# Mixture-of-experts kernel: 128-row tiles of one expert become two 64-row halves with an expert each, on two column tiles, in native fp32

## What is computed

```python
x = attn_out.transpose(0, 2, 1, 3).reshape(1152, 512)
# layer 0: 8 experts, w1[e] 512 x 1024, w2[e] 1024 x 512
expert_idx = argmax(x @ w_gate, 1); gate_w = softmax(...)[expert_idx]
y = gate_w * (relu(x @ w1[e]) @ w2[e])     # rows beyond the capacity of 288: zero
# layer 1: the same with weights of its own, for rows with y @ w_skip > 0
out = y.copy(); out[active] = y[active] + gate2_w * (relu(y @ w1[e]) @ w2[e])
```

## Times and profile before

| | |
|---|---|
| median of 3 executions | 707.31 us (703.5 to 710.21) |
| the profiled execution's own time | 709.03 us |
| its span | 707.3 us |
| PE busy | 640.4 us (91%) |
| PE weight loads busy | 453.4 us (64%) |
| DVE / ACT / POOL busy | 295.6 / 262.5 / 232.3 us |
| chain that ended last, by engine | PE 84%, DMA 4%, DVE 4% |

### The profile page before, as it was taken

How to read it: one execution, slowest core, us unless ns; L and a number is a source line. 1 busy time by engine, 2 the same in 40 slices (tenths; PEclk the granted TensorE clock), 3 DMA queues, 4 the chain that set the end, 5 groups by cost and what they waited for, 6 DMA issues and landing times.

```text
span 707.3 us, 11546 instructions
## 1 busy us (share of the span) xinstructions
PE 640.4 (91%) x3400; PEld 453.4 (64%) x3401; DVE 295.6 (42%) x501; ACT 262.5 (37%) x434; POOL 232.3 (33%) x211
## 2 busy tenths in 40 slices
PE   3759999999999999479999999999758999999984
PEld 3647877777777877356666766666456666566641
DVE  5426565666666574755303330120075654400000
ACT  4525565656565565222322322322202222222320
POOL 4173470825436830011211121121110444343332
PEclk9979999999999999789999999999959999999996
DMA  4786527163453104489912986140049999512110
GB/s 100 169 280 137 126 65 151 51 133 85 98 133 68 33 0 137 139 330 416 403 41 85 294 310 228 50 158 21 28 151 346 405 354 321 201 45 73 33 59 23
DMA packets 43446, 111.00 MB, mean 157 GB/s; under 512 B 16516, under 2 KB 16516, under 8 KB 42480
## 3 DMA queue, kind: packets, MB, share of 16 engines
q1 hardware_dynamic: 38384, 96.67, 43.3%
q0 software_dynamic: 5040, 14.06, 5.9%
HBM read 102.16 MB, written 13.37 MB: 163 GB/s over the span
## 4 chain that ended last, share of the span: by engine, by line
PE 84%; DMA 4%; DVE 4%; issue 3%; POOL 2%; ACT 2%; SPq 1%; ACTq 0%; POOLq 0%; DVEq 0%
PE psum L951 23%; PE psum L906 13%; PE psum L682 12%; PE psum L696 10%; PE psum L730 8%; PE psum L914 6%; PE psum L882 4%; PE psum L758 2%; DMA qraw<-in_q_dram 2%; PE psum L936 1%; DMA xraw<-moe_in,rows_in 1%; PE psum L742 1%; DMA wsecond<-in_moe_w_dram 1%; PE psum L887 1%; PE psum L726 1%
## 5 line engine op out<-in xcount | busy, mean ns | idle before, releaser
L951 PE MATMUL psum<-wsecond,HT 128*128 x384 | 175.8, 602 | 5.2 <-ACT HT L1119 4.6
L1182 DVE TENSOR_SCALAR_CACHE_REDUCE probs<-psum 128x1152 f32<-128x1152 f32 x72 | 97.6, 1357 | 75.2 <-PE psum L682 75.2
L951 PEld LDWEIGHTS psum<-wsecond,HT 128*128 128x128 f32 x384 | 72.1, 193 | 84.3 <-issue 83.4
L682 PE MATMUL psum<-KT,QT 128*128 128x384 f32 x480 | 106.6, 363 | 20.5 <-DVE KT L1289 9.8
L996 ACT ACTIVATE probs<-probs,nmax 128x1152 f32<-128x1152 f32 x72 | 90.7, 1260 | 48.3 <-DVE probs L1182 48.3
L682 PEld LDWEIGHTS psum<-KT,QT 128*128 128x128 f32 x480 | 84.9, 198 | 31.8 <-issue 16.6
L1339 DVE CAST wring<-wraw 128x1024 f32 (+1 forms) x56 | 39.9, 728 | 144.5 <-PE psum L914 136.3
L906 PE MATMUL psum<-wring,XTh 128*128 x384 | 98.2, 409 | 1.9 <-ACT XTh L1106 1.9
L696 PE MATMUL psum<-ident,probs 128*128 128x128 f32 x648 | 82.7, 276 | 3.3 <-ACT probs L996 2.8
L906 PEld LDWEIGHTS psum<-wring,XTh 128*128 128x128 f32 x384 | 72.5, 194 | 18.5 <-issue 2.8
L696 PEld LDWEIGHTS psum<-ident,probs 128*128 128x128 f32 x648 | 73.6, 142 | 11.5 <-issue 3.7
(11 more groups left out here) (163 smaller groups left out, 619.5 us busy)
## 6 DMA issues: line engine op xcount, KB each, us to landing
wraw<-in_moe_w_dram SPq DMA_DIRECT2D x64, 512.0 KB, 6.6
wsecond<-in_moe_w_dram SPq DMA_DIRECT2D x64, 512.0 KB, 7.8
qraw<-in_q_dram SPq DMA_DIRECT2D x30, 288.0 KB, 7.2
kraw<-in_k_dram SPq DMA_DIRECT2D x14, 576.0 KB, 7.2
V<-in_v_dram SPq DMA_DIRECT2D x8, 576.0 KB, 3.8
moe_in<-zero SPq DMA_DIRECT2D x9, 256.0 KB, 3.0
out_dram<-moe_in SPq DMA_DIRECT2D x1, 2304.0 KB, 9.6
moe_in<-xpair SPq DMA_DIRECT2D x16, 128.0 KB, 2.0
```

The source lines that it names most:

```text
L682: mm = pe.matmul(dst, QT[par][:, piece, q0:q0 + P], KT[par][:, b * S + c * KB:b * S + (c + 1) * KB], start=(i == 0), stop=(i == 2 * len(pa ...
L951: mm = pe.matmul(bank(Y_BANK), HT[:, c * P:(c + 1) * P], w, start=(c == 0), stop=(c == FC - 1), skip_group_check=True)
L1182: nc.vector.tensor_scalar(probs[:, t, :].rearrange("p (c k) -> p c k", c=3), scores_in(h, t), -SCALE, None, ALU.mult, ALU.min, accum_out=n ...
```

## The change

- **Tiles.** The unit is a grain of 64 rows (`GRAIN`); a tile is two grains, each with an expert of its own (`tab_grain`, one entry per grain). Experts begin on 64-row borders. `NSLOT`, the largest number of tiles, goes from 16 to 14.
- **Products.** `product` issues two matmuls with 64-column stationaries: the left grain into psum rows 0 to 63, moving the weights out of the ring, and the right grain into rows 64 to 127, moving a copy of its weights out of `wright`. Both products are native fp32. The cuts of W1 and X, `by_hi`, `by_lo`, `rest_of_x` and `cut_expert` go.
- **Copies.** `fill_right` copies the right grain's weights, 4 parts of 128 x 1024, for every tile: W1 on ACT, between relu(t) and the XT copy of tile t+1; W2 on DVE, right after `copy_y`.
- **Rings.** W1 4 experts, W2 3 experts (`RINGS`). SP's loop now issues W2 of expert a and then W1 of expert a+1, both waiting for the tiles of expert a-3: W2 for `y_done`, W1 for `hidden_done`.
- **Results.** The gate goes into relu's scale. DVE instead of ACT evacuates y; in layer 1 it adds the residual in the same instruction, so that it waits for `res_loaded` there, and `load_residual(t)` waits for `y_copied` of t-1. The logits of layer 1 are made by DVE, nine multiply-and-add reductions over 512 columns per tile with output to psum; only the last tile's go over PE as before.
- XT and HT are copied in halves; the constants of the subtraction go; three attention buffers move so that the rings fit; `wnext` (gate rows, broadcast to 128 partitions) is loaded once.

```diff
-    RING, RING2 = 2, 4
+    NTAB = NSLOT * PER_TILE
+    RINGS = (4, 3)
...
+        def fill_right(eng, copy, k, m, t, filled):
+            place = t * PER_TILE + 1
...
+            expert = eng.value_load(tab_grain[m][0:1, at], min_val=0, max_val=E - 1)
+            slot = eng.snap(ring_slot(k, m, expert))
+            for part in range(PARTS):
+                eng.wait_ge(w_loaded[k][part], expert * 16 + (E * m + 1) * 16)
+                copy(wright[k][:, part * PIECE:(part + 1) * PIECE],
+                     piece_of(k, slot, part).rearrange("p o f -> p (o f)")).then_inc(filled, 1)
...
+            def other_experts(m):
+                with sp.Fori(RINGS[1], E - 1) as a:
+                    load_second(m, a, m, a - RINGS[1])
+                    load_first(m, a + 1, m, a - RINGS[1])
+                load_second(m, E - 1, m, E - 1 - RINGS[1])
...
                 def load_residual(t, count):
+                    wait(pool, y_copied, t)
...
+                def product(k, lhs, b, c, cols, slot, first, last):
+                    left = wring[k][:, bass.ds(slot, 1), cols].rearrange("p o f -> p (o f)")
+                    pe.matmul(psum[0:GRAIN, b, :], lhs[:, c * P:c * P + GRAIN], left, start=first, stop=last,
+                              skip_group_check=True)
+                    return pe.matmul(psum[GRAIN:P, b, :], lhs[:, c * P + GRAIN:(c + 1) * P], wright[k][:, cols],
+                                     start=first, stop=last, skip_group_check=True)
...
-                def step(t, first=False, second=False):
-                    ring = first_weights(t)
-                    pe.wait_ge(xt_ready, t + 1)
-                    by_hi(XTh, (HID_BANK, HID_BANK + 1), DC, F, ring)
...
-                    by_lo(XTl, (HID_BANK, HID_BANK + 1), DC, F, ring).then_inc(hidden_done, 1)
+                def step(t, first=False):
+                    hidden_product(t)
+                    if first:
+                        pe.wait_ge(gates_found, m + 1)
+                    else:
+                        y_product(t - 1)
                     turn_x(t + 1)
...
-                        next_logits(t - 2)
                     turn_hidden(t)
...
+                def step(t):
                     relu(t)
+                    act.wait_ge(hidden_done, t + (START + 1))
+                    fill_right(act, nc.scalar.copy, FIRST, m, t + 1, w1_right_[m])
                     copy_xt(t + 1)
+                    copy_hidden(t)
...
+            def copy_y(m, t):
+                dve.wait_ge(y_done_[m], t + (START + 1))
+                wait(dve, y_stored_[m], t * 16)
+                if m == 0:
+                    nc.vector.tensor_copy(ysb[:], bank(Y_BANK)).then_inc(y_copied_[m], 1)
+                else:
+                    dve.wait_ge(res_loaded, 16 * t + 16)
+                    nc.vector.tensor_tensor(orow[:], bank(Y_BANK), res[:], ALU.add).then_inc(y_copied_[m], 1)
+            def next_logits(t):
+                dve.wait_ge(y_copied_[0], t + 1)
+                for e in range(E + 1):
...
+                    nc.vector.tensor_tensor_reduce(out=bank((YT_BANK, LG_BANK)[e % 2]), in0=ysb[:], in1=wnext[:, e, :], scale=1.0, scalar=0.0,
+                                                   op0=ALU.mult, op1=ALU.add, accum_out=lrow[:, e:e + 1]
+                                                   ).then_inc(lrow_ready, 1)
...
+                def step(t):
+                    copy_y(m, t)
+                    fill_right(dve, nc.vector.tensor_copy, SECOND, m, t + 1, w2_right_[m])
+                    if m == 0:
...
+                        next_logits(t)
```

More of the change, by code:

```diff
@@ new lines, in hidden_product @@
+                def hidden_product(t):
+                    expert = left_expert(t)
+                    slot = pe.snap(ring_slot(FIRST, m, expert))
+                    wait(pe, relu_ready, t)
+                    for c in range(DC):
+                        pe.wait_ge(w_loaded[FIRST][c], expert * 16 + (E * m + 1) * 16)
+                        pe.wait_ge(w1_right_[m], PARTS * t + (c + 1))
+                        if c % 2 == 0:
+                            pe.wait_ge(xt_ready, 2 * t + (1 + c // 2))
+                        for i in range(F // 512):
+                            mm = product(FIRST, XT, HID_BANK + i, c, slice(c * F + i * 512, c * F + (i + 1) * 512), slot,
+                                         c == 0, c == DC - 1)
+                    mm.then_inc(hidden_done, 1)
@@ new lines, in y_product @@
+                def y_product(t):
+                    expert = left_expert(t)
+                    slot = pe.snap(ring_slot(SECOND, m, expert))
+                    wait(pe, y_copied, t)
+                    for c in range(FC):
+                        part = c // (FC // PARTS)
+                        if c % (FC // PARTS) == 0:
+                            pe.wait_ge(w_loaded[SECOND][part], expert * 16 + (E * m + 1) * 16)
+                            pe.wait_ge(w2_right_[m], PARTS * t + (part + 1))
+                        if c % (FC // 2) == 0:
+                            pe.wait_ge(ht_ready, 2 * t + (1 + c // (FC // 2)))
+                        mm = product(SECOND, HT, Y_BANK, c, slice(c * DM, (c + 1) * DM), slot, c == 0, c == FC - 1)
+                    mm.then_inc(y_done, 1)
@@ L977, in _ @@
                 turn_x(0)
                 step(0, first=True)
-                step(1, second=True)
+                step(1)
                 with pe.Fori(2, NSLOT) as t:
@@ L1129, in copy_yt @@
-                def copy_yt(t):
-                    act.wait_ge(y_turned, t + 1)
-                    nc.scalar.copy(yT[:], bank(YT_BANK)).then_inc(yt_ready, 1)
-                def copy_logits(t):
-                    act.wait_ge(lg_done, t + 1)
-                    at = slice(t, t + 1) if isinstance(t, int) else bass.ds(t, 1)
-                    nc.scalar.copy(logits2[:, at, :].rearrange("p o c -> p (o c)"), bank(LG_BANK, E + 1)
-                                   ).then_inc(lg_copied, 1)
-                def step(t, first=False, second=False):
-                    if not first:
-                        copy_hidden(t - 1)
+                    for i in range(2):
+                        act.wait_ge(hid_turned, 2 * t + (i + 1))
+                        if i == 0:
+                            wait(act, y_done_[m], START + t)
+                        nc.scalar.copy(HT[:, i * 512:(i + 1) * 512], bank(HT_BANK + i)).then_inc(ht_ready, 1)
```

423 lines of the change are left out of this document (152 added, 271 removed).

## The result

| | before | after |
|---|---|---|
| median | 708.76 us (703.5 to 710.69, 4 executions) | 719.95 us (718.86 to 721.92, 4 executions) |
| ratio, with 95% interval | 1 | 1.0152 (1.0115 to 1.0188) |
| span of the profiled execution | 707.3 us | 717.1 us (its own time 718.86) |

What follows compares the result with a forecast made beforehand. PE was taken to bound both tile loops. Layer 0 -39.9, routing +0.3, layer 1 +31.6 and tail -2.6 summed to -10.6 on 707.3, so 697 us; own range 683 to 711, wider 672 to 716.

Steps and rivals of the forecast that it cites:

- the price of the waits in layer 1: Layer 1's late W1 loads put at 33.6 us and late residual gathers at 14.9, giving layer 1 199.6 us, +31.6.
- The tile on PE: Both tile loops: 10 and 9 tiles, 15.2 us of PE per step, each pair of passes 0.43 us.
- column tiles don't overlap: Rival in the tile products: paired passes lack full overlap, 13.7 us more per tile, 958 us; chance 0.06.
- The logit reductions: DVE's nine per tile, put at 0.8 us each, 7.2 us; DVE 11.1 of 15.2 us per tile, hidden.
- that rival (718 us): DVE becomes the bound of layer 0, from 1.25 us per reduction, 718 us at 1.44; chance 0.12.
- Layer 0: The first layer's tile loop: 166.5 us against 206.4, a gain of 39.9 us.
- Weights late in layer 1: W1 of experts 5 and 6 13.8 us late ahead of tiles 3 and 4, plus 3.0 clock each: 33.6 us.
- the weights come in time: Rival in layer 1: W1 loads of experts 5 and 6 not late, 33.6 us go, 663 us; chance 0.12.
- Residual late: Layer 1: DVE's copy_y waits for the residual gather, with W2's fill behind it; 14.9 us in all.
- The total: Whole span: -39.9 + 0.3 + 31.6 - 2.6 = -10.6 us on 707.3, so 697 us.
- Everything in layer 1 a bit worse: Rival of worse clock and gathers in layer 1, counted inside the forecast's own range, without a chance of its own.

Runs made afterwards that it cites:

- the short loops: e7 with the tile loops of PE, ACT, DVE and POOL ending at these inputs' 10 and 9 tiles: 641.7 us, ratio 0.9064 to the kernel before.
- e6: e3 with ACT copying XT of tile 1 before filling W1's right half in each layer's first step: 649.09 us, ratio 0.914 to the kernel before.
- e2: Changed kernel with POOL gathering the residual one step earlier, behind the store of tile t-1: 693.29 us, ratio 0.9777 to the kernel before.
- e3: Changed kernel with both edits, W1 issued before W2 and the residual gathered a step earlier: 658.28 us, ratio 0.9292 to the kernel before.
- e5: Changed kernel with DVE only copying y out in layer 1 and POOL adding the residual, gather as late as before: 699.03 us (one execution).
- e7: e6 with SP issuing W1 loads one expert further ahead, W1 of a+2 before W2 of a: 646.27 us, ratio 0.9087 to the kernel before.
- e1: Changed kernel with SP issuing W1 of expert a+1 before W2 of expert a: 695.47 us, ratio 0.9812 to the kernel before.
- e8: e3 with experts beginning on 128-row borders again, 13 and 11 tiles, both halves of a tile the same expert: 729.11 us (one execution).
- e4: Changed kernel, same load order, with W2 of experts 3 to 6 of layer 1 loaded by half: 714.56 us (one execution).

## Why the prediction was wrong

The step that failed is the price of the waits in layer 1. The waits that were named are the ones that came, but W1 late by 13.8 us was 16.7 and 17.2, the gathers put at 14.9 us in all took 19.8, and the lower clock behind a gather's wait, which the working put at nothing without a reason, took 4.3 more. Layer 1 came out at 215.6 us and not 199.6, and that is 16.0 of the 20.4 us by which the span was missed.

**The tile on PE: right.** 10 and 9 tiles. A pair of passes starts every 0.43 us, 32 pairs in a row, and a step takes 352.36 - 337.01 = 15.35 us, against 15.2. PE's timeline in after, layer 0, one step:

```profile
337.01 0.64 PE L887 MATMUL psum<-w1ring,XT 128*64 x1
337.02 0.64 PE L889 MATMUL psum<-wright,XT 128*64 128x512 f32 x1
337.50 0.59 PE L887 MATMUL psum<-w1ring,XT 128*64 x1
...
337.92 0.59 PE L887 MATMUL psum<-w1ring,XT 128*64 x1
...
343.93 0.59 PE L887 MATMUL psum<-w2ring,HT 128*64 x1
```

The left and the right half start within 0.01 us of each other. First product 6.92, y product 6.87, turns 1.56: of the 1.48 that I had put for turns and for going in and out of column tiles, 0.08 were missing. The rival "column tiles don't overlap" (958 us) is out; attention's rows were a sound basis for 64 passes in a row. The Trainium skill (TensorEngine Tiling (Array Packing), Key Properties) says that a change of tiling mode drains TensorE. The trace doesn't show a drain by itself, but it bounds the price: the turns of 128 x 128 between the products, with a change of mode on either side, take 1.56 us, against 0.44 + 0.79 of the earlier trace rows.

**DVE: right.** The logit reductions, in after, layer 0:

```profile
462.96 0.14 DVE L1281 DVE_READ_ACCUMULATOR2_ANT lrow<- 128x1 f32 x1
462.96 0.73 DVE L1281 CUSTOM_DVE_ANT_0 psum<-ysb,wnext 128x512 f32<-128x512 f32 x1
...
468.42 0.17 DVE L1286 COPY logits<-lrow 128x9 f32 x1
471.03 0.69 DVE L1271 COPY ysb<-psum 128x512 f32<-128x512 f32 x1 [2.43 <-issue]
```

0.73 us each and one every 0.65, under the 0.8 taken and far from the 1.25 at which that rival (718 us) decides. Its 718 is near the measured time, by luck: DVE is busy for 85.75 of the 169.90 us of layer 0.

**Layer 0: the mechanism right, 3.4 us short.** The first product has 9.15 us instead of 8.4 (+0.75); the gap to tile 1 is 5.9, not 5.5 (+0.4), but the clock costs 1.6 there, not 3.0 (-1.4); steps and the gap ahead of y(9) +1.0; from the end of y(9) to the routing 6.9 instead of 4.2 (+2.7). The last is a step that the working left out: DVE leaves its loop only after the skipped tiles, and copies y(9) 2.9 us after it is done, where 0.7 was put. With the short loops it is 0.97 us.

**Weights late in layer 1: right in place and cause, too small.** Two gaps, ahead of tiles 3 and 4, released by ACT's copies waiting for W1, just as named. The order of SP's loop removed both and the bytes hardly mattered, so the rival "the weights come in time" (663 us) is out. The term that was mis-sized is the wait: 13.8 us each were put, 16.7 and 17.2 measured (+6.3 in all). At tile 3, SP asks 0.9 us after y(1) ends (0.3 was put), the last part is copied 15.7 us after SP's first issue (13.6 was put for bytes, landing, gathers and store), and 1.7 us lie from there to the first pass (1.45 was put). The clock took 2.3 and 2.0 instead of 3.0 each (-1.7).

**Residual late: right in kind, too small.** The experiments with an early gather and with POOL's addition both removed it. Put were 14.9 us: y(1) 5.0, y(4) 2.5, y(5) to y(7) 0.9 each, y(8) 4.7. Measured: 6.1, 3.7, 1.4 to 1.5 each, and for y(8) 0.8 more than the gap that the working gave it (10.0 against 9.2), so 19.8: +4.9. The failed part is that these waits cost clock too: +2.6 at y(1) and +1.7 at y(4). I had counted the clock for the 14 us gaps and for the loop ends only, though the row of an idle time of 3.08 us with its 3 us of loss was in hand. A wait of 3.6 or 5.9 us should have had the same surcharge.

The sum for layer 1: W1 gaps +6.3 and -1.7, gathers +4.9 and +4.3, eight steps +1.2, the gap to tile 1 +0.6, together +15.6 of the +16.0 measured.

**The total.** -39.9 for layer 0 against +31.6 for layer 1 left -10.6. Measured are -36.5 and +47.6. Each of the layers is off by less than a tenth of its length, but the difference changed its sign: nothing that I named was absent, nothing big was unnamed, and nearly all misses went the same way, because waits were costed without what follows on a wait (the clock, the loop's exit) and the burst as if the DMA were full from the start. "Everything in layer 1 a bit worse" stood in the text as part of the forecast's own range, 683 to 711, and was not worked out. With the text's own upper bounds it comes to 711.4: 3.1 more for each landing, 2.5 for y(4)'s gather and 3.0 of clock at y(1) and y(4). That passes the range's 711 and is still short of the 717.1 measured.

## What to carry to other kernels

When two experts share a tile, every load has a new deadline: for each load, look up which wait stands ahead of it in the queue that issues it, and whether that wait is really about this load's own buffer; here two exchanged lines were worth 24 us, and the order was wrong because W1 of expert 5 is needed by the first product of tile 3, W2 of expert 4 only by y(3), a step later. A copy on which PE depends must not stand behind a wait for a gather in the same engine's queue; gather earlier or let another engine wait. And where a change is a large gain less a large loss, put the surcharges (clock, loop exit, last copy) on each wait before taking the difference.

## What the runs showed of the hardware

**The clock after short waits.** Idle time of PE before a product (the figure in brackets in its row), and how much longer that product took than the 6.92 us of a first and the 6.87 of a second product, from PE's timelines of the changed kernel and all experiments:

| idle | extra time of the product | where |
|---|---|---|
| 0.8 to 1.4 us | 0.1 at most | among others e6 (503.59), after (649.01) |
| 2.1 us | 0.05 in three kernels, 1.75 in two | last y product of e2, e3, e5; of e6, e7 |
| 2.5 us | 0.0 | e6, tile 3 |
| 2.9 us | 1.6 | e3, tile 3 |
| 3.4 to 3.7 us | 1.5 to 2.9 | tile 1 in after, e1 to e5 and e8, y(4) in after, e1, e4 |
| 4.5 us | 1.6 | y(1) in e1 and e4 |
| 5.7 to 5.9 us | 2.1 to 2.6 | after, y(1); e1, y(2) and y(3) |
| 8.4 us | 1.5 to 3.0 | last y of after, e1, e4 |
| 14.4 to 17.6 us | 1.4 to 3.0 | tiles 3 and 4 of after, e2, e4, e5 |

(e1 is W1 first, e2 the early gather, e3 both together, e4 half of W2, e5 POOL's addition, e6 XT first, e7 W1 two ahead, e8 no shared tiles.) The first product of a layer is left out: it follows on the routing, in which PE works less (in after 8.24 of 19.40 us ahead of layer 1), and takes 1.4 to 3.0 us longer with only 0.9 to 2.9 us of idle time just before it. The same idle time with and without the loss, last y product of both together and of XT first:

```profile
642.28 0.64 PE L888 MATMUL psum<-w2ring,HT 128*64 x1 [2.12 <-DVE wright L313]
```
```profile
631.07 1.06 PE L888 MATMUL psum<-w2ring,HT 128*64 x1 [2.11 <-DVE wright L313]
```

At 2.1 us the loss came in two kernels of five; in every row of 2.9 us of idle time or more it came, in most of them from the first pass on (1.11 us, the lower level of 1.2 GHz), and the price hardly grows with the wait: never over 3.0 us. What decides at 2.1 us stays open. A gap of 3.6 us may cost nearly as much again in clock. The Trainium skill (TensorE: Matmul & The Clock Gate, Part 1) says that how many matmuls run at the lower level differs from run to run of one kernel; the traces fit that: tile 1 of layer 0, where the edit of e2 doesn't act yet, took 1.5 us more in the one and 2.9 in the other, after the same 3.36 us of idle time.

**A skipped iteration isn't free.** Four skipped tiles cost DVE 2.43 - 0.18 = 2.25 us, 0.56 each (W1 two ahead against the short loops), and they lay on the path, since the last tile's work stands behind the loop.

**A gather beside a burst.** A gather of 128 rows of 512 fp32 took 8.6 us from issue to use while weights loaded (529.15 to 537.75 in after), and 3.7 in quiet (685.86 to 689.60 with POOL's addition).
